# Block attention and two gated layers on one core: value sums copied in three pieces, C21 activated first, and masking with its maximum as one VectorE operation per head pair

## The chip, the cores and the metric

The kernel runs on one core of a Trainium2 chip. Five engines work side by side, each on its own list of instructions in order, and wait for one another on semaphores: TensorE (PE, matmuls into the accumulation memory, `ps`), VectorE (DVE), ScalarE (ACT), GpSimd (POOL) and SyncE (SP, which here only issues DMAs). DMAs are issued on two queues, one of SP (q1 in the profile) and one of ACT (q10). The metric is the device time of one execution in microseconds; lower is better.

## The reference, cut to what matters

Attention over 2 batches, 8 heads, 768 positions, head width 64. A query sees the keys less than 16 positions away, and beside them 24 summaries, one for every block of 32 keys; the attention output goes through a gated layer and then a second layer.

```
k_sum = k by blocks of 32: maximum;   v_sum = v by blocks of 32: mean
scores_l = scale * q k^T,  -1e9 where |i - j| >= 16
scores_s = scale * q k_sum^T + log(32)
a = softmax over [scores_l, scores_s];  x = a @ [v, v_sum]
g = x @ w_gate;  y = (g * sigmoid(g) * (x @ w_val)) @ w_out
h = y @ w_in;    out = where(h >= 1, h, where(h <= -1, 0, (h + 1)^2 / 4)) @ w_out2
```

## The kernel before, in words

**Attention tiles.** Queries are handled in 24 tiles `s` of 64 positions, 12 of each batch. A tile takes all 8 heads as 4 head pairs, 128 partitions (64 positions of each of two heads) by 128 columns a pair: 96 keys in and around the tile, 24 summaries, 8 columns of padding. For each tile:

- PE: `scores(s)` (L486).
- DVE: `mask_scores(s)`: a first instruction (L1050) reads the scores of all four pairs from `ps`, 128x512, multiplies by the scale, adds the mask and writes `masked`. A second one (L1053) reads `masked` back and writes the four negated maxima to `neg_max`. Between the two it waits for its own semaphore `masked_ready`; ACT waits for the second (`max_ready`).
- ACT: `exponentials(s)` (L773): one activation for each head pair, with the negated maximum as bias, and the row sum as a second output, which shows in the profile as an instruction of its own (ACTIVATION_READ_ACCUMULATOR).
- DVE: `inverses(s)` (L1059, L1061); POOL: `normalise(s)` (L1335); PE: `transposes` (L493); ACT: `copy_trans` (L784); PE: `values` (L514), whose right operand `v_s` has 96 rows of values and under them 32 rows of value sums; the result is copied to `raw` by DVE (first batch, `first_copy_out`, L1065) or ACT (second batch).

**The first batch** (`LAST_A` = 12 tiles, up to about 57 us) runs as a pipeline: at step `s` PE does the scores of `s`, the transposes of `s-3` and the values of `s-7` (`VLAG`). At steps 3 to 5 it also makes the value sums (L471), which ACT copies to `v_sum` (L749). `place_first_sums` then puts them under the values of all 12 tiles: tiles 0 and 1 by one activation (L752), tiles 2 to 11 by one DMA on ACT's queue (L755, 640 KB). PE waits for that DMA (`v_first_sums`) before the values of tile 2. The values themselves, the keys of the second batch (`k_raw_b`) and weights come on SP's queue at the same time. DVE also makes the low part of weight unit 0: `w_lo_a(0)` and `w_lo_b(0)` (L1115, L1125) at step 1 and `w_lo_s(0)` (L1120) at step 4.

**The second batch's 12 tiles** are woven into phase 0 of the layers, one tile for each unit `u` (about 70 to 175 us).

**The layers.** Each product is done in three matmuls of high and low parts (L524), with the matrix cut 2x2 and seven block products a unit; `c11`, `c12`, `c21`, `c22` are the blocks of the result. In phases 0 and 1 even units are gates, odd ones values. For a gate, ACT takes C21 out of `ps` to `silu[:, 3]` (L871), then `silu_c11` (L879), and `silu_rest`: first blocks 1 and 2 in one activation (L883, after `c12_ready` of DVE), then C21 (L885). The value unit's `h21` on DVE (L1151) multiplies C21 and frees the bank for the first product (`p1`) of the unit after next; POOL multiplies the other blocks (L1345). Phases 2 and 3 are the second layer.

**Order.** Nothing is scheduled by a planner: each engine's order is the order of the calls in the code.

Of the kernel before, what the change touches and what calls it, by code (L numbers as in the profile page):

```python
# [9 lines left out]
ACT = mybir.ActivationFunctionType  # L10
ALU = mybir.AluOpType
AX = mybir.AxisListType

P = 128
B, H, S, D = 2, 8, 768, 64
BLOCK, WINDOW = 32, 16
SCALE = 1.0 / math.sqrt(D)
MASKED = -1e9
DM = H * D
TOK = B * S  # L20
KD = DM // P
PAIRS = H // 2

QT = 64
TILES = S // QT
G = B * TILES
SUB = 16
WIN = QT + 2 * WINDOW
NB = S // BLOCK
COLS = 128  # L30
# [5 lines left out]
RING = 4  # L36
# [31 lines left out]
LAST_A = G // 2  # L68
FIRST = TILES // 2
VLAG = 7  # L70

def phase_of(u):
# [31 lines left out]
def build(nc, q_t, k_t, v_rows, w1, w2, out):  # L105
    ctx = ExitStack()
    with ctx:
# [3 lines left out]
        def sem(name):  # L111
            return ctx.enter_context(nc.semaphore(name))
# [14 lines left out]
        part = at("part", 112640, [2, 3, T])  # L127
        silu = at("silu", 121856, [4, T])
# [3 lines left out]
        v_s = at("v_s", 128000, [TILES, DM])  # L132
# [14 lines left out]
        v_sum = at("v_sum", 193536, [B, DM])  # L147
        masked = at("masked", 197632, [2, PAIRS, COLS])
# [3 lines left out]
        mask = at("mask", 207872, [2 * MASKS, COLS])  # L152
        ident = at("ident", 210944, [P])
        k_sum = at("k_sum", 211456, [B, 2, PAIRS, SUB])
        neg_max = at("neg_max", 212480, [RING, PAIRS])
# [16 lines left out]
        def score_banks(s):  # L172
            b = 0 if s < LAST_A and s % 2 == 0 else AT0
            return ps[:, b:b + 2, 0:2 * COLS]
# [45 lines left out]
        def prob_of(s):  # L220
            return prob_s[:, s % RING] if s < LAST_A else prob[:, s % 2]
# [16 lines left out]
        qk_loaded = [sem(f"qk_loaded{j}") for j in range(6)]  # L238
        v_first_loaded = [sem(f"v_first_loaded{j}") for j in range(FIRST)]
        v_pair_sums = sem("v_pair_sums")  # L240
        v_first_sums = sem("v_first_sums")
        v_late_loaded = [sem(f"v_late_loaded{j}") for j in range(2)]
        v_late_sums = [sem(f"v_late_sums{j}") for j in range(2)]
        scores_done = sem("scores_done")
        masked_ready = sem("masked_ready")
        max_ready = sem("max_ready")
        exp_done = sem("exp_done")
        denom_ready = sem("denom_ready")
        inv_ready = sem("inv_ready")
# [32 lines left out]
        c21_act = sem("c21_act")  # L282
        c21_dve = sem("c21_dve")
        silu_c11_ready = sem("silu_c11_ready")
        silu_ready = sem("silu_ready")
        h_pool = sem("h_pool")

# [174 lines left out]
        def _(pe):  # L462
# [33 lines left out]
            def values(s, dst):  # L496
                v, c0 = v_slots(s // 2)
                r = c0 + s % 2
                if s % 2 == 0:
                    pr = s // 2  # L500
                    pe.wait_ge(v_first_loaded[pr] if pr < FIRST else v_late_loaded[pr % 2], v_count(pr))
                    if s == 0:
                        pe.wait_ge(v_pair_sums, 1)
                    elif s == 2:
                        pe.wait_ge(v_first_sums, 16)
                    if pr in (FIRST, FIRST + 1):
                        pe.wait_ge(v_late_sums[pr % 2], 16)
                pe.wait_ge(prob_t_ready, s + 1)
                for x in range(2):
                    for half, row in ((0, 0), (1, 1), (1, 0), (0, 1)):  # L510
                        i = 2 * row + x
                        a = pair_at(i, half)
                        c = (2 * a + row) * D
                        last = nc.tensor.matmul(dst[row * D:row * D + D, a], v[:, r, c:c + D],  # L514
                                                prob_t_of(s)[:, i, half * QT:half * QT + QT], start=True, stop=True)
                last.then_inc(attn_done, 1)
# [184 lines left out]
            for k in range(PHASES):  # L701
                u1 = PH_U0[k] + PH_LEN[k] - 1
                for r in range(PH_LEN[k]):
                    u = PH_U0[k] + r
# [41 lines left out]
        def _(act):  # L746
# [4 lines left out]
            def place_first_sums():  # L751
                nc.scalar.activation(v_s[WIN:, 0:2], v_sum_ps[0][WIN:, :].unsqueeze(1).to_broadcast([P - WIN, 2, DM]),  # L752
                                     ACT.Copy).then_inc(v_pair_sums, 1)
                act.wait_ge(v_sum_ready, 1)
                act.dma_start(v_s[WIN:, 2:], v_sum[WIN:, 0].unsqueeze(1).to_broadcast([P - WIN, TILES - 2, DM])  # L755
                              ).then_inc(v_first_sums, 16)

            def place_late_sums(j):
                act.wait_ge(v_sum_ready, 2)
# [2 lines left out]
                              ).then_inc(v_late_sums[j], 16)  # L762

            def exponentials(s):
                act.wait_ge(max_ready, s + 1)
                if s < LAST_A:
                    if s >= RING:
                        act.wait_ge(trans_done, s - RING + 1)
                elif s >= LAST_A + 2:
                    act.wait_ge(trans_done, s - 1)  # L770
                c = s % RING
                for a in range(PAIRS):
                    last = nc.scalar.activation(prob_of(s)[:, a], masked[:, s % 2, a], ACT.Exp,  # L773
                                                bias=neg_max[:, c, a:a + 1], accum_out=total[:, c, a:a + 1])
                last.then_inc(exp_done, 1)

# [102 lines left out]
                nc.scalar.activation(silu[:, 0], part[:, u % 2, 0], ACT.Silu).then_inc(silu_c11_ready, 1)  # L879

            def silu_rest(u):
                act.wait_ge(c12_ready, u + 1)
                nc.scalar.activation(silu[:, 1:3], part[:, u % 2, 1:3], ACT.Silu)  # L883
                act.wait_ge(c21_act, u // 2 + 1)
                nc.scalar.activation(silu[:, 3], silu[:, 3], ACT.Silu).then_inc(silu_ready, 1)  # L885

            def wout_part_hi(k, i):
# [142 lines left out]
        def _(dve):  # L1031
# [10 lines left out]
            def mask_scores(s):  # L1042
                t = s % TILES
                m = 0 if t == 0 else MASKS - 1 if t == TILES - 1 else 1
                dve.wait_ge(scores_done, s + 1)
                if s >= 2:
                    dve.wait_ge(exp_done, s - 1)
                rows = mask[:, 2 * m:2 * m + 2].rearrange("p x c -> p (x c)").unsqueeze(1)
                rows = rows.to_broadcast([P, 2, 2 * COLS])
                nc.vector.scalar_tensor_tensor(masked[:, s % 2].rearrange("p (b x) c -> p b (x c)", b=2), score_banks(s),  # L1050
                                               SCALE, rows, ALU.mult, ALU.add).then_inc(masked_ready, 1)
                dve.wait_ge(masked_ready, s + 1)
                nc.vector.tensor_reduce(neg_max[:, s % RING], masked[:, s % 2], AX.X, ALU.max, negate=True  # L1053
                                        ).then_inc(max_ready, 1)

            def inverses(s):
                c = s % RING
# [89 lines left out]

            def h21(u):
                dve.wait_ge(p4_done, u + 1)
                dve.wait_ge(silu_ready, u // 2 + 1)  # L1150
                nc.vector.tensor_tensor(h[:, chunks_of(u)[1], 0:T], x_ps(u), silu[:, 3], ALU.mult).then_inc(c21_dve, 1)  # L1151

# [34 lines left out]
            for j in range(P // BLOCK):  # L1188
                last = nc.vector.memset(sel[j * BLOCK:(j + 1) * BLOCK, SEL0 + j:SEL0 + j + 1], 1.0 / BLOCK)
            last.then_inc(sel_ready, 1)  # L1190
            nc.vector.memset(mask[:, :, WIN:WIN + NB], math.log(BLOCK))
            nc.vector.memset(mask[:, :, WIN + NB:], MASKED)
            nc.vector.memset(half[:], 0.5).then_inc(half_ready, 1)
            nc.vector.memset(k_sum[:, :, 1, :, NB - SUB:], 0.0).then_inc(pads_ready, 1)
# [10 lines left out]
            for s in range(LAST_A):  # L1205
                mask_scores(s)
                if s >= 1:
                    inverses(s - 1)
                if s > VLAG:
                    first_copy_out(s - VLAG - 1)  # L1210
                if s == 1:
                    w_lo_a(0)
                    w_lo_b(0)
                elif s == 4:
                    w_lo_s(0)
# [194 lines left out]
```

## Time and profile before

| | us |
|---|---|
| median of three runs | 624.05 (623.77 to 625.68) |
| profiled execution, its own time | 624.35 |
| its span, first to last instruction | 622.5 |
| PE busy in the span | 588.6 (95%) |
| DVE busy | 479.6 (77%) |
| ACT busy | 365.0 (59%) |
| mean granted TensorE clock | 0.994 |

The span is what the trace shows; the 1.85 us by which the execution's time exceeds it lie around it. PE is busy nine tenths or more of nearly every fortieth from the sixth on; the forty slices show it idle in the first four or five (2, 9, 5, 8, 8 tenths), which are the first batch's attention. So this is a kernel bound by PE for most of its length, with a short first stage in which PE waits.

### The profile page before, as it was taken

What the parts mean: (1) busy time and instruction counts of PE and PEld (TensorE: products, weight loads), DVE (VectorE), ACT (ScalarE), POOL (GpSimd) and SP (SyncE); (2) the same over time, 40 slices, a digit from 0 to 9 for tenths busy, and PEclk for the clock granted to TensorE, in tenths of its full rate; (3) what the DMA queues carried; (4) which work ended last, traced back from release to release, by engine and by line L of the source; (5) the groups of instructions that cost most, each with busy time, mean ns of one, the idle gap of its engine ahead of it and who ended that gap; (6) DMA issues with size and microseconds to landing.
All of it is one profiled execution on the core that took longest, in us unless ns stands there. A gap on an engine that the chain in (4) does not pass through costs nothing.

```text
span 622.5 us, 10059 instructions
## 1 busy us (share of the span) xinstructions
PE 588.6 (95%) x3720; PEld 538.7 (87%) x3720; DVE 479.6 (77%) x770; ACT 365.0 (59%) x735; POOL 87.2 (14%) x78
## 2 busy tenths in 40 slices
PE   2958889999999999999999999999999999999997
PEld 2436679888889999999999999999878899998886
DVE  6649698899858656888867756997998569979843
ACT  3845687887865536555554536666565356665532
POOL 4425032324330001222320000000000000000000
PEclk9979999999999999999999999999999999999999
DMA  9968333425112211223222112322212233012212
GB/s 332 308 180 274 99 111 119 131 66 187 35 53 74 63 34 41 93 72 102 85 68 70 51 35 69 113 74 68 68 52 67 102 103 97 23 35 67 68 51 102
DMA packets 32928, 59.77 MB, mean 96 GB/s; under 512 B 3248, under 2 KB 7344, under 8 KB 32880
## 3 DMA queue, kind: packets, MB, share of 16 engines
q1 hardware_dynamic: 32384, 58.21, 29.3%
q10 hardware_dynamic: 496, 0.92, 0.6%
q8 instruction: 30, 0.49, 0.3%
q14 instruction: 18, 0.15, 0.1%
HBM read 54.53 MB, written 3.15 MB: 93 GB/s over the span
## 4 chain that ended last, share of the span: by engine, by line
PE 73%; DVE 13%; ACT 5%; issue 4%; DMA 3%; POOL 1%; SPq 0%; ACTq 0%; POOLq 0%; DVEq 0%
PE ps L524 38%; PE ps L661 17%; PE ps L633 15%; DMA v_s<-v_sum 2%; PE ps L486 1%; ACT prob L773 1%; DVE hid_lo L1163 1%; ACT L879 1%; DVE masked L1050 1%; DVE w_sum L1107 1%; DVE w_sum L1109 1%; DMA k_a<-k_t_dram 1%; PE ps L493 1%; DVE rel L1169 1%; PE ps L471 1%
## 5 line engine op out<-in xcount | busy, mean ns | idle before, releaser
L524 PE MATMUL ps<-x_hi,w_hi 128*128 128x384 f32 x560 | 191.2, 341 | 5.7 <-DVE h L1151 3.1
L524 PE MATMUL ps<-x_lo,w_hi 128*128 128x384 f32 x560 | 187.4, 335 | 0.0
L524 PE MATMUL ps<-x_hi,w_lo 128*128 128x384 f32 x560 | 187.2, 334 | 0.0
L524 PEld LDWEIGHTS ps<-x_hi,w_hi 128*128 128x128 f32 x560 | 105.1, 188 | 10.2 <-issue 4.9
L524 PEld LDWEIGHTS ps<-x_hi,w_lo 128*128 128x128 f32 x560 | 105.2, 188 | 0.4 <-issue 0.2
L524 PEld LDWEIGHTS ps<-x_lo,w_hi 128*128 128x128 f32 x560 | 105.1, 188 | 0.0
L893 ACT ACTIVATE wout_hi<-wout_raw 128x512 fp32r<-128x512 f32 x56 | 35.3, 631 | 95.1 <-PE ps L661 52.0
L661 PE MATMUL ps<-wout_hi,hid_hi 128*128 128x512 f32 x192 | 74.8, 389 | 0.8 <-DVE wout_lo L1157 0.8
L661 PE MATMUL ps<-wout_hi,hid_lo 128*128 128x512 f32 x192 | 75.2, 392 | 0.1
L661 PE MATMUL ps<-wout_lo,hid_hi 128*128 128x512 f32 x192 | 74.8, 390 | 0.0
L1157 DVE TENSOR_TENSOR wout_lo<-wout_raw,wout_hi 128x512 fp32r<-128x512 f32 x56 | 39.4, 704 | 40.1 <-ACT wout_hi L893 39.6
L1345 POOL TENSOR_TENSOR h<-part,silu 128x384 f32<-128x384 f32 x36 | 47.7, 1333 | 138.1 <-ACT silu L885 90.6
L633 PE MATMUL ps<-hid_lo,wout_hi 128*128 128x384 f32 x192 | 64.5, 336 | 0.6 <-DVE hid_lo L1163 0.6
L633 PE MATMUL ps<-hid_hi,wout_hi 128*128 128x384 f32 x192 | 64.3, 335 | 0.7 <-DVE wout_lo L1157 0.7
L633 PE MATMUL ps<-hid_hi,wout_lo 128*128 128x384 f32 x192 | 64.1, 334 | 0.0
L1120 DVE TENSOR_TENSOR w_lo<-w_sum,w_hi 128x1024 fp32r<-128x1024 f32 x40 | 48.8, 1220 | 19.3 <-ACT w_hi L829 19.3
L1163 DVE TENSOR_TENSOR hid_lo<-h,hid_hi 128x768 fp32r<-128x768 f32 x56 | 53.5, 956 | 1.4
L906 ACT ACTIVATE hid_hi<-h 128x768 fp32r<-128x768 f32 x56 | 46.6, 832 | 2.4 <-DVE h L1172 2.4
L829 ACT ACTIVATE w_hi<-w_sum 128x1024 fp32r<-128x1024 f32 x40 | 42.2, 1055 | 7.4 <-PE ps L524 5.1
L661 PEld LDWEIGHTS ps<-wout_hi,hid_lo 128*128 128x128 f32 x192 | 36.0, 188 | 8.5 <-DVE hid_lo L1163 1.2
L661 PEld LDWEIGHTS ps<-wout_hi,hid_hi 128*128 128x128 f32 x192 | 36.0, 188 | 8.4 <-issue 1.1
L661 PEld LDWEIGHTS ps<-wout_lo,hid_hi 128*128 128x128 f32 x192 | 36.0, 188 | 7.5
(105 smaller groups left out, 920.1 us busy)
## 6 DMA issues: line engine op xcount, KB each, us to landing
w_raw<-w_dram SPq DMA_DIRECT2D x80, 256.0 KB, 2.9
wout_raw<-w_dram SPq DMA_DIRECT2D x56, 256.0 KB, 2.6
out_dram<-y_out SPq DMA_DIRECT2D x12, 256.0 KB, 2.1
k_a<-k_t_dram SPq DMA_DIRECT2D x6, 384.0 KB, 6.8
v_s<-v_rows_dram SPq DMA_DIRECT2D x6, 384.0 KB, 14.8
v_a<-v_rows_dram SPq DMA_DIRECT2D x6, 384.0 KB, 3.7
k_raw<-k_t_dram SPq DMA_DIRECT2D x3, 512.0 KB, 4.5
q_a<-q_t_dram SPq DMA_DIRECT2D x6, 256.0 KB, 6.5
```

The lines of the kernel that those rows point to most:

```text
L471: last = nc.tensor.matmul(v_sum_ps[b][:], sel[:, c0:c0 + P], v_tok[b][:, i], start=i == 0, stop=i == VCH - 1)
L486: last = nc.tensor.matmul(dst[half * QT:half * QT + QT, row, x * COLS:x * COLS + COLS], q[rows, r, a], k[rows, r, :, a], start=True, stop= ...
L524: last = nc.tensor.matmul(dst, lhs, rhs, start=start and kk == 0 and i == 0, stop=kk == 1 and i == 2, skip_group_check=not start)
L633: last = nc.tensor.matmul(bank[ACC1[j]][:, 0:T], lhs, rhs, start=i == 0 and e == 0, stop=ends and e == 2)
L661: last = nc.tensor.matmul(bank[ACC2[j]][:], lhs, rhs, start=i == 0 and e == 0, stop=ends and e == 2)
L829: nc.scalar.activation(w_hi[:, u % 2, W_S2:W_S4 + 1], w_sum[:], ACT.Copy).then_inc(ws_hi, 1)
L893: nc.scalar.activation(wout_hi[:, n % 2], wout_raw[:, n % RAWS], ACT.Copy).then_inc(wout_hi_ready, 1)
L906: nc.scalar.activation(hid_hi[:, n % 2], h[:, c], ACT.Copy).then_inc(hid_hi_ready, 1)
L1120: nc.vector.tensor_tensor(w_lo[:, u % 2, W_S2:W_S4 + 1], w_sum[:], w_hi[:, u % 2, W_S2:W_S4 + 1], ALU.subtract).then_inc(ws_lo, 1)
L1157: nc.vector.tensor_tensor(wout_lo[:, n % 2], wout_raw[:, n % RAWS], wout_hi[:, n % 2], ALU.subtract).then_inc(wout_lo_ready, 1)
L1163: nc.vector.tensor_tensor(hid_lo[:, n % 2], h[:, c], hid_hi[:, n % 2], ALU.subtract).then_inc(hid_lo_ready, 1)
L1345: nc.gpsimd.tensor_tensor(dst, part[:, u % 2, c], silu[:, c], ALU.mult).then_inc(h_pool, 1)
```

## The change

Four edits:

1. `place_first_sums` issues three DMAs in place of one: tiles 2 and 3, tiles 4 to 7, tiles 8 to 11 (128, 256 and 256 KB), each with its own semaphore. PE waits for the first before the values of tile 2, for the second before those of tile 4, for the third before those of tile 8.
2. `mask_scores` does for each of the four head pairs one `tensor_tensor_reduce` of 128x128: (score + mask) times minus the scale, written to `masked`, and its minimum to `neg_max` as a second output. `masked` is thus negated, the exponential takes it with scale -1, and the mask's log(32) is divided by the scale. `max_ready` is gone; ACT waits for `masked_ready`, which now comes after the last pair.
3. `silu_rest` activates C21 first, with a semaphore of its own (`silu_c21_ready`) that `h21` waits for; then blocks 1 and 2.
4. `w_lo_a(0)` and `w_lo_b(0)` stand at step 3 in place of step 1.

```diff
+SUMS_AT = ((2, 4), (4, 8), (8, TILES))
@@ values, on PE
-                    elif s == 2:
-                        pe.wait_ge(v_first_sums, 16)
+                    for j, (c0, _) in enumerate(SUMS_AT):
+                        if s == c0:
+                            pe.wait_ge(v_first_sums[j], 16)
@@ place_first_sums, on ACT
-                act.dma_start(v_s[WIN:, 2:], v_sum[WIN:, 0].unsqueeze(1).to_broadcast([P - WIN, TILES - 2, DM])
-                              ).then_inc(v_first_sums, 16)
+                for j, (c0, c1) in enumerate(SUMS_AT):
+                    act.dma_start(v_s[WIN:, c0:c1], v_sum[WIN:, 0].unsqueeze(1).to_broadcast([P - WIN, c1 - c0, DM])
+                                  ).then_inc(v_first_sums[j], 16)
@@ exponentials, on ACT
-                act.wait_ge(max_ready, s + 1)
+                act.wait_ge(masked_ready, s + 1)
-                    last = nc.scalar.activation(prob_of(s)[:, a], masked[:, s % 2, a], ACT.Exp,
+                    last = nc.scalar.activation(prob_of(s)[:, a], masked[:, s % 2, a], ACT.Exp, scale=-1.0,
@@ silu_rest, on ACT
+                act.wait_ge(c21_act, u // 2 + 1)
+                nc.scalar.activation(silu[:, 3], silu[:, 3], ACT.Silu).then_inc(silu_c21_ready, 1)
                 act.wait_ge(c12_ready, u + 1)
-                nc.scalar.activation(silu[:, 1:3], part[:, u % 2, 1:3], ACT.Silu)
-                act.wait_ge(c21_act, u // 2 + 1)
-                nc.scalar.activation(silu[:, 3], silu[:, 3], ACT.Silu).then_inc(silu_ready, 1)
+                nc.scalar.activation(silu[:, 1:3], part[:, u % 2, 1:3], ACT.Silu).then_inc(silu_ready, 1)
@@ mask_scores, on DVE
-                rows = mask[:, 2 * m:2 * m + 2].rearrange("p x c -> p (x c)").unsqueeze(1)
-                rows = rows.to_broadcast([P, 2, 2 * COLS])
-                nc.vector.scalar_tensor_tensor(masked[:, s % 2].rearrange("p (b x) c -> p b (x c)", b=2), score_banks(s),
-                                               SCALE, rows, ALU.mult, ALU.add).then_inc(masked_ready, 1)
-                dve.wait_ge(masked_ready, s + 1)
-                nc.vector.tensor_reduce(neg_max[:, s % RING], masked[:, s % 2], AX.X, ALU.max, negate=True
-                                        ).then_inc(max_ready, 1)
+                rows = mask[:, 2 * m:2 * m + 2]
+                for i in range(PAIRS):
+                    last = nc.vector.tensor_tensor_reduce(
+                        masked[:, s % 2, i], score_banks(s)[:, i // 2, i % 2 * COLS:i % 2 * COLS + COLS], rows[:, i % 2],
+                        -SCALE, 3e38, ALU.add, ALU.min, neg_max[:, s % RING, i:i + 1])
+                last.then_inc(masked_ready, 1)
@@ h21, on DVE
-                dve.wait_ge(silu_ready, u // 2 + 1)
+                dve.wait_ge(silu_c21_ready, u // 2 + 1)
@@ on DVE, before the tiles
-            nc.vector.memset(mask[:, :, WIN:WIN + NB], math.log(BLOCK))
+            nc.vector.memset(mask[:, :, WIN:WIN + NB], math.log(BLOCK) / SCALE)
@@ the first batch's steps, on DVE
-                if s == 1:
+                if s == 3:
                     w_lo_a(0)
                     w_lo_b(0)
```

DVE, steps 1 and 2 of the first batch, before (masking of tile 1, inverses of tile 0, low weight parts, masking of tile 2, with what each waits for):

```order
L1050 SCALAR_TENSOR_TENSOR masked<-ps,mask 128x512 [waits scores_done]
L1053 TENSOR_REDUCE neg_max<-masked 128x4 [waits masked_ready]
L1059 TENSOR_SCALAR denom<-total 128x4 [waits exp_done]
L1061 RECIPROCAL inv<-denom 128x4 [waits denom_ready]
L1115 TENSOR_TENSOR w_lo<-w_raw,w_hi 128x512 [waits wa_hi]
L1125 TENSOR_TENSOR w_lo<-w_raw,w_hi 128x256 [waits wb_hi]
L1050 SCALAR_TENSOR_TENSOR masked<-ps,mask 128x512 [waits exp_done,scores_done]
```

DVE, the same place now: the inverses of tile 0, the masking of tile 2, and the inverses of tile 1:

```order
L1061 TENSOR_SCALAR denom<-total 128x4 [waits exp_done]
L1063 RECIPROCAL inv<-denom 128x4 [waits denom_ready]
L1053 ISA masked,neg_max<-ps,mask 128x128 [waits exp_done,scores_done]
L1053 ISA neg_max 128x1
L1053 ISA masked,neg_max<-ps,mask 128x128
L1053 ISA neg_max 128x1
...
L1061 TENSOR_SCALAR denom<-total 128x4 [waits exp_done]
L1063 RECIPROCAL inv<-denom 128x4 [waits denom_ready]
```

A tile's masking, two instructions before, is eight now: four of 128x128 and behind each one that writes its second output, 128x1. None of the eight waits for DVE itself. The two `w_lo` instructions stand two steps later.

ACT at steps 5 and 6, before (copy of the value sums, their placing under tiles 0 and 1, the DMA for tiles 2 to 11, then the copy of tile 3's transposes and the exponentials of tile 6):

```order
L749 ACTIVATE v_sum<-ps 32x512 [waits v_sum_done]
L752 ACTIVATE v_s<-ps 32x1024
L755 DMA v_s<-v_sum 32x10x512 [waits v_sum_ready]
L784 ACTIVATE prob_ts<-ps 128x512 [waits trans_done]
L773 ACTIVATE prob_s,total<-masked,neg_max 128x128 [waits trans_done,max_ready]
```

ACT, the same place now:

```order
L751 ACTIVATE v_sum<-ps 32x512 [waits v_sum_done]
L754 ACTIVATE v_s<-ps 32x1024
L758 DMA v_s<-v_sum 32x2x512 [waits v_sum_ready]
L758 DMA v_s<-v_sum 32x4x512 x2
L787 ACTIVATE prob_ts<-ps 128x512 [waits trans_done]
L776 ACTIVATE prob_s,total<-masked,neg_max 128x128 [waits trans_done,masked_ready]
```

Three issues stand where one did, ahead of everything that ACT does for the tiles from 3 on; the rest of its order is the same up to the gates' `silu_rest`.

## Rows read from the trace of the kernel before

**Rows 1.** The page: PE's busy tenths in 40 slices, and the chain that ended last.

```profile
PE   2958889999999999999999999999999999999997
...
PE 73%; DVE 13%; ACT 5%; issue 4%; DMA 3%; POOL 1%; SPq 0%; ACTq 0%; POOLq 0%; DVEq 0%
```

**Rows 2.** Stretches: us, busy of PE, PEld, DVE, ACT, POOL, PEclk, DMA share, GB/s.

```profile
33.70:41.10 7.40, 0.00 (x0) 0.03 (x1) 1.46 (x5) 2.83 (x14) 1.37 (x2) 0.76 0.99 283
41.10:44.30 3.20, 3.20 (x38) 2.42 (x38) 0.92 (x2) 0.00 (x0) 0.00 (x0) 0.50 0.04 18
...
47.90:62.00 14.10, 12.71 (x145) 8.66 (x143) 13.96 (x23) 6.61 (x18) 8.05 (x7) 1.00 0.92 296
```

**Rows 3.** PE in time order: start, us, line, out<-in, count, idle before.

```profile
31.59 0.69 PE L514 MATMUL ps<-prob_ts,v_s 128*64 128x64 f32 x16
32.21 0.67 PE L486 MATMUL ps<-k_a,q_a 64*64 64x128 f32 x16
33.03 0.66 PE L493 MATMUL ps<-ident,prob_s 128*128 128x128 f32 x4 [0.15 <-ACT prob_ts L784]
41.10 1.12 PE L514 MATMUL ps<-prob_ts,v_s 128*64 128x64 f32 x16 [7.42 <-DMA v_s<-v_sum]
```

**Rows 4.** ACT's DMA queue from 31.4 to 33.4 us; the DMA's size and landing.

```profile
q10 hardware_dynamic: 37, 0.08, 16.7%
...
v_s<-v_sum ACTq DMA_DIRECT2D x1, 640.0 KB, 13.4
```

**Rows 5.** ACT in time order, 27 to 68 us.

```profile
27.44 0.72 ACTq L755 DMA_DIRECT2D v_s<-v_sum  x1
...
36.33 0.20 ACT L773 ACTIVATION_READ_ACCUMULATOR prob_s<-masked,neg_max 128x1 f32 x1
44.36 0.60 ACT L784 ACTIVATE prob_ts<-ps 128x512 f32<-128x512 f32 x1 [7.83 <-PE ps L493]
...
67.52 0.49 ACT L859 ACTIVATE part<-ps 128x384 f32<-128x384 f32 x1 [1.38 <-issue]
```

**Rows 6.** The second batch's keys: issues (ns, first and last start), and landing.

```profile
L340 SPq DMA_DIRECT2D k_raw_b<-k_t_dram x3: 515/734/1120, 22.4 to 24.2; - x3
...
DMA to landing us min/median/max: 18.2/18.3/18.9
```

**Rows 7.** DVE in time order, first batch: a copy, the masking behind it, key maxima.

```profile
32.83 0.39 DVE L1065 COPY raw<-ps 128x256 f32<-128x256 f32 x1
33.14 0.68 DVE L1050 SCALAR_TENSOR_TENSOR masked<-ps,mask 128x512 f32<-128x512 f32 x1
...
47.93 1.21 DVE L1035 TENSOR_REDUCE k_sum<-k_raw_b 128x32 f32<-128x1024 f32 x1
```

**Rows 8.** ACT in time order: an exponential, the read of its sum, the next.

```profile
29.22 0.39 ACT L773 ACTIVATE prob_s<-masked,neg_max 128x128 f32<-128x128 f32 x1
29.51 0.19 ACT L773 ACTIVATION_READ_ACCUMULATOR prob_s<-masked,neg_max 128x1 f32 x1
29.61 0.39 ACT L773 ACTIVATE prob_s<-masked,neg_max 128x128 f32<-128x128 f32 x1
```

**Rows 9.** POOL in time order: the normalisations of tiles 0 and 1.

```profile
13.69 1.40 POOL L1335 TENSOR_TENSOR prob_s<-prob_s,inv 128x512 f32<-128x512 f32 x1 [0.59 <-DVE inv L1061]
17.06 1.04 POOL L1335 TENSOR_TENSOR prob_s<-prob_s,inv 128x512 f32<-128x512 f32 x1 [1.97 <-DVE inv L1061]
```

**Rows 10.** DVE in time order, in phase 0: masking, low weight part, h21.

```profile
107.12 0.67 DVE L1050 SCALAR_TENSOR_TENSOR masked<-ps,mask 128x512 f32<-128x512 f32 x1
107.83 0.69 DVE L1053 TENSOR_REDUCE neg_max<-masked 128x4 f32<-128x512 f32 x1
108.43 0.68 DVE L1115 TENSOR_TENSOR w_lo<-w_raw,w_hi 128x512 fp32r<-128x512 f32 x1
109.03 0.55 DVE L1151 TENSOR_TENSOR h<-ps,silu 128x384 f32<-128x384 f32 x1
```

**Rows 11.** Who waited for whom, 75 to 220 us: total us, times, longest.

```profile
PE ps L524 <- DVE h L1151: 3.1, 5, 0.9
```

More of the change, by code:

```diff
@@ L240, in build @@
         v_pair_sums = sem("v_pair_sums")
-        v_first_sums = sem("v_first_sums")
+        v_first_sums = [sem(f"v_first_sums{j}") for j in range(len(SUMS_AT))]
         v_late_loaded = [sem(f"v_late_loaded{j}") for j in range(2)]
@@ L245, in build @@
         masked_ready = sem("masked_ready")
-        max_ready = sem("max_ready")
         exp_done = sem("exp_done")
@@ L284, in build @@
         silu_c11_ready = sem("silu_c11_ready")
+        silu_c21_ready = sem("silu_c21_ready")
         silu_ready = sem("silu_ready")
```

## The prediction

> **What bounds the kernel now.** I read the page's forty slices and chain first, then the stretches, then PE's, ACT's and DVE's rows in time order around the edits, and last the waits. The chain is PE for 73% of the span, and PE is nine tenths busy or more in every slice from the seventh to the last but one [rows 1]. There an edit on another engine can hardly gain. What the change can move lies in the first batch's attention, in the slices before, and in phase 0 as far as PE waits there.
>
> The one large hole: PE would start the values of tile 2 behind the transposes at 33.03 + 0.66 = 33.7 us, and starts them at 41.10, after 7.42 us of waiting for the DMA of the value sums [rows 3]. ACT has nothing to do from 36.5 to 44.36 us [rows 5]. The wait hurts twice: the granted clock is 0.50, TensorE's lower level of 1.2 GHz, for the 3.2 us behind it, after an engine that had been idle [rows 2].
>
> **Three pieces.** The DMA is issued at 27.44 [rows 5] and takes 13.4 us to land, to 40.85 [rows 4]. Until 33.4 us its queue has moved 37 packets, 0.08 of the 0.64 MB, all behind 31.4 [rows 4]; an eighth of the way is done at 33.4, so the first packets leave at some 32.5, and the whole takes 8.4 us beside SP's transfers. Ahead of the first piece's end lie only its own bytes, a fifth: 32.5 + 0.2 x 8.4 = 34.2, and up to a microsecond for the slowest of 16 engines and the semaphore. I take 35.2. The second piece ends at three fifths, about 38, the third at about 41.
>
> What it adds: two issues on ACT, ahead of all that ACT does from tile 3 on. The two later issues of this kind held ACT up for 1.38 us with work behind them [rows 5]; I take 1.3. From there to 36.5 us ACT has nearly no gap, and PE waits for ACT's copies (0.15 us ahead of the transposes at 33.03 [rows 3]), so PE comes to the values of tile 2 at up to 34.9 in place of 33.7. That lies inside the wait for the piece. The values start at R = 35.2.
>
> What is late next is ACT itself. Its exponentials of tile 9 end at 36.5 [rows 5], now at 37.8. The transposes that it needs then are ready 0.69 + 0.67 + 0.66 us behind R at full clock [rows 3], at 37.2. So its copy starts at 37.8 in place of 44.36 [rows 5], 6.55 us sooner. From there to tile 11 a few tenths of waiting for PE at half clock and for DVE go too: 6.7 in all. A tile costs ACT four times 0.39 [rows 8] and a copy of 0.60 [rows 5], about 2 us, so tile 4's values are wanted at R + 4 = 39 and tile 8's behind 43: neither waits for its piece.
>
> Then DVE's copies and key maxima. The first maxima start at 47.93 [rows 7], now at 41.2. Their keys, issued from 22.4 on, take 18.3 us: the first third is there at 40.7, the last at 24.2 + 18.9 = 43.1 [rows 6]. The cover is half a microsecond. From 47.9 to 62 us DVE is busy 13.96 of 14.1 us [rows 2], so that stretch just moves forward. Term: **-6.7 us**, with ends -7.4 (the whole wait) and -4 (pieces or keys late, below).
>
> **Low weight parts two steps later.** At step 1 they stood ahead of tile 2's masking and beside POOL's first normalisation, which took 1.40 us against the next one's 1.04 [rows 9], and PE's first transposes wait for it. They hide behind DVE's wait for scores at step 4; without that cover they cost what they cost before. PE's chain starts up to 0.36 us earlier, which does not reach the landing of the piece if SP's backlog sets that. Between 0 and -0.36: **-0.1**.
>
> **Masking.** Before: two instructions, 1.31 us from the start of the masking to the start of what follows (107.12 to 108.43) [rows 10]. Now four of 128x128 out of `ps` and four that write a second output. No row shows either. A copy of 128x256 out of `ps` takes 0.31 us start to start [rows 7], a reduction of 128x512 0.60 [rows 10]; the line through them gives 0.165 for 128 columns, and by the durations, 0.39 and 0.69, it gives 0.24. The nearest row for a second output is ACT's: the read starts 0.29 us behind the exponential, the next exponential 0.10 behind the read, so a pair takes no longer than the exponential's own duration, 0.39 [rows 8]. Carried over: 0.24 a pair, 0.97 a tile. If the read costs its 0.19 whole on top of 0.165, it is 1.42 a tile; if nothing overlaps (0.24 + 0.19), 1.7; with a free read, 0.66. I take 1.2, between the two middle readings: 0.1 less than before.
>
> The Trainium skill, VectorE: DVE Perf Modes, Rules for kernel authors, speaks against this edit: chained operations should not be fused for speed, the number of operations should be kept down. Here the columns read are halved and two instructions become eight, so by that rule the tile would get slower and by the estimate a little faster; no row of before decides it.
>
> It counts where PE waits for DVE. In phase 0 PE waits five times, 3.1 us in all, 0.9 once and so 0.55 each otherwise, for `h21` [rows 11], which stands right behind masking and `w_lo` [rows 10]. A tenth less on DVE is a tenth less on PE in six pairs of units: **-0.6 us**, with ends -2.7 (free read: of 3.1 nearly all) and +6 (1.7 a tile, in the way of the third rival). In the first batch DVE's tile hides behind ACT's 2 us. `masked_ready` comes later for PE than before, at the end of all four pairs, but PE asks for it a step later: nothing.
>
> **C21 first.** `h21` stands on DVE behind masking and `w_lo`, when C21 is long activated, so PE's waits for it [rows 11] end on DVE's own order. In phase 1 there are none of them in the list, and PE's work hides what ACT gains: **0**.
>
> **Sum.** -6.7 - 0.1 - 0.6 = -7.4 on the profiled execution: span 622.5 to 615.1, and with the 1.85 us around it 624.35 to 616.95. It lies 0.3 above the median of the runs, so 624.05 - 7.4 = **616.65 us**. A difference within 0.3% (1.9 us) is called no change, about what a measurement of this kernel can tell.
>
> **Rivals.** *The next transfer takes the wait's place.* The first piece or the keys land late, since the 16 DMA engines are 0.99 busy [rows 2]. At R = 38 ACT's copy starts at 40, 4.4 us sooner, and the sum is about -5: 619.1. For it: half a microsecond of cover at the keys. Against: bytes and order are the same.
>
> *The second output is nearly free.* 0.66 to 0.97 a tile, 0.65 to 0.34 less than before in six pairs, as far as there is wait to take: -2 to -2.7 in place of -0.6, 614.5 to 615.3. For it: ACT's pair takes no longer than its exponential [rows 8].
>
> *The second output drains the engine.* This is the other side: a pair takes 0.6 us, 2.4 a tile, 1.1 more than before. Phase 0 pays it in each of six pairs of units ahead of `h21`, and again ahead of the next exponentials, which start the other tile's way to DVE: 12 x 1.1 = 13.2. In the first batch DVE's tile (2.4 + 0.31 for a copy, and the inverses) passes ACT's 2 us, some +3 from tile 8 on. 624.05 - 6.8 + 16.2 = 633.5. It eats half the gain from 0.38 us a pair on and turns the sign at about 0.45. Against: that is nearly twice a 128-column duration.
>
> *The change doesn't do what it says.* The three pieces land together at 41. Then the wait stays and hides ACT's two issues: 623.5. Against: the pieces have a semaphore each and follow one another on one queue.
>
> **How the numbers follow.** Forecast 0.62 (615.3 to 618). Late transfers 0.15 (618 to 621). Nearly free output 0.13 (614.5 to 615.3). Dear output 0.07, of which 0.04 slower than before. No use of the pieces 0.03. The range, 614.6 to 620.6, leaves out the ends of these, under 2 in 10. Faster 0.92, no change 0.04, slower 0.04.
>
> **What would show it.** PE's wait for `v_s` between 33 and 41 us shrinks to under 2 us, and the granted clock stays at 2.4 GHz behind it. ACT shows three issues and then runs without a gap to tile 11. The second batch's first key maxima start at about 41. In phase 0 PE's waits for `h21` shrink by a tenth each, and a tile's eight instructions take 1.0 to 1.4 us. It would be wrong if the key maxima start after 43, or if the eight take over 1.6 us.

## The result and the profile after

```
                          before   after
median of the runs, us    624.87   614.01   (after 613.82 to 615.82, 4 runs; before 623.77 to 626.07)
profiled execution, us             614.17
span, us                  622.5    612.4
first key maxima, us       47.93    41.10
first h21, us              89.72    81.47
a pair of units, us        19.31    18.84
```

The ratio is 0.9832, with an interval of 0.9803 to 0.9861. The prediction was 616.65 us, range 614.6 to 620.6; the time lies 2.6 us under it and 0.6 us under the range.

The page of the kernel after, first PE's and the clock's slices and the chain, which answer to [rows 1]:

```profile
PE   2889999999999999999999999999999999999997
...
PEclk9989999999999999999999999999999999999999
...
PE 80%; DVE 9%; SPq 3%; DMA 3%; issue 2%; ACT 2%; POOL 0%; ACTq 0%; POOLq 0%; DVEq 0%
```

PE is 80% of the chain instead of 73%. The 5 in its third slice has gone, and the row of nines begins in the fourth slice instead of the seventh. DMA still has 3%, now by the second batch's keys.

PE in time order at the start of the first batch (start, us, line, out<-in, count, idle before), which answers to [rows 3]:

```profile
28.42 1.12 PE L494 MATMUL ps<-ident,prob_s 128*128 128x128 f32 x4 [2.36 <-ACT prob_ts L787]
29.46 1.12 PE L516 MATMUL ps<-prob_ts,v_s 128*64 128x64 f32 x16
...
34.72 0.66 PE L494 MATMUL ps<-ident,prob_s 128*128 128x128 f32 x4
35.30 0.69 PE L516 MATMUL ps<-prob_ts,v_s 128*64 128x64 f32 x16
```

No row here waits for `v_s`. The values of tile 2 start at 35.30 us, not 41.10. But PE waited 2.36 us for ACT at 28.42, and from there its groups take 1.12 us instead of 0.66 to 0.69. The stretches show the clock (us, busy of PE, PEld, DVE, ACT, POOL, PEclk, DMA share, GB/s), and answer to [rows 2]:

```profile
27.40:34.20 6.80, 5.78 (x68) 4.56 (x72) 1.85 (x13) 5.62 (x24) 2.08 (x2) 0.53 1.07 265
34.20:41.10 6.90, 6.40 (x122) 4.80 (x116) 5.01 (x35) 6.35 (x30) 3.12 (x3) 0.97 1.05 298
41.10:55.20 14.10, 12.48 (x139) 8.42 (x135) 13.96 (x22) 6.24 (x16) 7.46 (x6) 1.00 0.94 307
```

Over 6.8 us the mean granted clock is 0.53, so nearly all of the stretch is at the lower level of 1.2 GHz (0.50). Ahead of it stood the 2.36 us without work. What PE waited for shows on ACT, in time order, which answers to [rows 5], and in the landing of the three pieces, which answers to [rows 4]:

```profile
25.37 2.35 ACTq L758 DMA_DIRECT2D v_s<-v_sum  x3
27.77 0.60 ACT L787 ACTIVATE prob_ts<-ps 128x512 f32<-128x512 f32 x1 [1.52 <-issue]
...
35.41 0.60 ACT L787 ACTIVATE prob_ts<-ps 128x512 f32<-128x512 f32 x1 [0.55 <-PE ps L494]
...
DMA to landing us min/median/max: 8.0/9.4/10.4
```

The three issues hold ACT for 2.35 us. The first piece, issued at 25.37, is there 8.0 us later, at 33.4. By then the values of tile 2 are still behind the slow groups on PE, so nobody waits for it. The DVE rows of the second batch's keys answer to [rows 7]:

```profile
41.10 1.22 DVE L1038 TENSOR_REDUCE k_sum<-k_raw_b 128x32 f32<-128x1024 f32 x1 [0.48 <-DMA k_raw_b<-k_t_dram]
...
42.86 1.19 DVE L1038 TENSOR_REDUCE k_sum<-k_raw_b 128x32 f32<-128x1024 f32 x1
...
47.22 1.20 DVE L1038 TENSOR_REDUCE k_sum<-k_raw_b 128x32 f32<-128x1024 f32 x1
```

```profile
80.02 0.28 DVE L1053 CUSTOM_DVE_ANT_0 masked<-ps,mask 128x128 f32<-128x128 f32 x1
80.23 0.08 DVE L1053 DVE_READ_ACCUMULATOR2_ANT neg_max<- 128x1 f32 x1
80.23 0.28 DVE L1053 CUSTOM_DVE_ANT_0 masked<-ps,mask 128x128 f32<-128x128 f32 x1
...
80.86 0.08 DVE L1053 DVE_READ_ACCUMULATOR2_ANT neg_max<- 128x1 f32 x1
80.86 0.68 DVE L1117 TENSOR_TENSOR w_lo<-w_raw,w_hi 128x512 fp32r<-128x512 f32 x1
81.47 0.55 DVE L1153 TENSOR_TENSOR h<-ps,silu 128x384 f32<-128x384 f32 x1
```

The read starts together with the next operation, each operation 0.21 us behind the last, and `w_lo` starts 0.84 us behind the masking. Before it was 1.31. The waits from 60 to 220 us (total us, times, longest), which answer to [rows 11]:

```profile
PE ps L526 <- ACT part L862: 1.4, 1, 1.4
PE ps L494 <- POOL prob L1337: 1.0, 1, 1.0
PE ps L635 <- DVE wout_lo L1159: 0.7, 1, 0.7
PE ps L526 <- DVE h L1153: 0.4, 1, 0.4
```

PE's waits for `h21` are down from 3.1 us in five to 0.4 in one.

**Where the 10.1 us of the span went.** Up to the first key maxima: 47.93 to 41.10, 6.83 us. From there to the first `h21`: 41.79 before, 40.37 after, 1.42 us. Over the four pairs of units that follow: 4 x 0.47 = 1.9 us. Together 10.1. And 1.42 is three times 0.47, the 1.31 - 0.84 of a tile: three tiles of the second batch are masked in this stretch, and in the kernel before PE waited for DVE behind each (the last row is the first of the five waits of [rows 11]):

```profile
72.79 0.41 PE L524 MATMUL ps<-x_hi,w_hi 128*128 128x384 f32 x1 [0.33 <-DVE part L1140]
...
79.48 0.44 PE L524 MATMUL ps<-x_hi,w_hi 128*128 128x384 f32 x1 [0.26 <-DVE w_lo L1115]
...
90.42 0.41 PE L524 MATMUL ps<-x_hi,w_hi 128*128 128x384 f32 x1 [0.92 <-DVE h L1151]
```

Two of these waits are shorter than 0.47 us, but the stretches between the same groups of PE bear the figure out. From 68.16 to 76.12, 82.87 and 90.42 it is 7.96, 6.75 and 7.55 us; in the kernel after, from 61.31 to 68.81, 75.08 and 82.16, it is 7.50, 6.27 and 7.08. Each is 0.46 to 0.48 us shorter. So seven tiles stand on PE's path, at 0.47 us each: 3.3 us. PE's waits say the same: 3.1 + 0.3 + 0.3 us before, 0.4 now.

### The profile page after: what moved, and what is told of

The parts are those of the page before. It is cut to its first block, busy times and chain, and to the rows that moved or that the text cites. A ratio compares the mean times of both kernels' runs of the same rounds, so it can differ in the third digit from the quotient of the medians.

```text
span 612.4 us, 10207 instructions
## 1 busy us (share of the span) xinstructions
PE 588.3 (96%) x3720; PEld 539.3 (88%) x3720; DVE 469.8 (77%) x914; ACT 365.1 (60%) x735; POOL 87.2 (14%) x78
## 4 chain that ended last, share of the span: by engine, by line
PE 80%; DVE 9%; SPq 3%; DMA 3%; issue 2%; ACT 2%; POOL 0%; ACTq 0%; POOLq 0%; DVEq 0%
PE ps L526 45%; PE ps L663 17%; PE ps L635 15%; DMA k_raw_b<-k_t_dram 3%; DVE hid_lo L1165 1%; SPq L380 1%; PE ps L516 1%; PE ps L487 1%; DVE rel L1171 1%; DVE x_lo L1097 1%; DVE h L1174 1%; SPq L359 1%; PE ps L494 1%; DVE t_first L1089 1%; DVE t_late L1089 1%
```

## Experiments

The times are medians in us; the ratios are against runs of the kernel before that were taken on the same chip in between.

```
kernel                   median  ratio   95% interval      span   first key  h21 waits
before                    624.9                            622.5   47.93     3.1, 5
after                     614.01 0.9832  0.9803 to 0.9861  612.4   41.10     0.4, 1
only pieces               618.26 0.9895  0.9882 to 0.9907  616.1   41.51     3.1, 5
only two-output masking   620.24 0.9922  0.9906 to 0.9937  618.8   47.46     0.4, 1
only C21 first            624.77 0.9998  0.9990 to 1.0007  623.3   48.65     3.1, 5
only w_lo later           623.79 0.9984  0.9975 to 0.9993  622.5   47.87     3.1, 5
after without pieces      619.09 0.9902  0.9882 to 0.9922  617.2   45.97     0.4, 1
after, masking of before  618.12 0.9886  0.9866 to 0.9906  616.2   41.69     3.1, 5
after, w_lo at step 1     614.10 0.9828  0.9813 to 0.9843  613.0   41.67     0.4, 1
after + DVE work          616.96 0.9874  0.9861 to 0.9888  614.5   40.67     2.5, 5
after, pieces later       614.77 0.9835  0.9822 to 0.9849  613.2   41.27     0.4, 1
same, keys first          612.86 0.9810  0.9797 to 0.9824  611.3   40.09     0.4, 1
after, keys first         613.76 0.9814  0.9790 to 0.9837  611.9   40.18     0.4, 1
```

### Each part alone

The diffs below are cut to the main lines of each edit.

**Three pieces only**, on the kernel before:

```diff
-                act.dma_start(v_s[WIN:, 2:], v_sum...).then_inc(v_first_sums, 16)
+                for j, (c0, c1) in enumerate(SUMS_AT):
+                    act.dma_start(v_s[WIN:, c0:c1], v_sum...).then_inc(v_first_sums[j], 16)
```

> The kernel before with the value sums in three pieces alone. Theory (the pieces give the first-stage term, masking gives the rest): the pieces are issued at 27.4 us, ACT is held up 1.3 to 1.5 us, tile 2's values start at about 35.3 to 36, the second batch's first key maxima at 41.2 to 42 in place of 47.9: 6.0 to 6.8 us less than before, and PE's waits for h21 in phase 0 stay at about 3.1 us. Rival (the pieces gain more than the rest lets be seen): 7.4 or more less.

618.26 us, 6.4 us off the span. The key maxima start at 41.51, and the `h21` waits are those of before. The pieces' term holds in size. PE's wait behind ACT's issues is there too (2.76 us ahead of the transposes at 30.10, and 1.12 us for the values behind; the kernel before has 1.27 us at this place), so it belongs to the pieces.

**Two-output masking only**, on the kernel before:

```diff
-                nc.vector.scalar_tensor_tensor(masked..., score_banks(s), SCALE, rows, ALU.mult, ALU.add)
-                nc.vector.tensor_reduce(neg_max..., masked..., AX.X, ALU.max, negate=True)
+                for i in range(PAIRS):
+                    last = nc.vector.tensor_tensor_reduce(masked..., score_banks(s)..., rows[:, i % 2],
+                        -SCALE, 3e38, ALU.add, ALU.min, neg_max[:, s % RING, i:i + 1])
```

> The kernel before with the masking as four two-output operations a tile alone. Theory (masking was mis-sized): a tile's masking takes 0.84 us in place of 1.31, PE's wait for h21 in phase 0 goes from 3.1 to under 0.6 us, and the time falls by 3 to 3.5 us; the wait for the value sums stays at about 7 us, a little longer since PE gets there sooner. Rival (C21 first is what ended the waits for h21): less than 1 us gained, waits for h21 still near 3.

620.24 us: the ratio gives 4.9 us (3.9 to 5.9), the span 3.7. Of the span 0.47 came ahead of the key maxima; from the maxima to the first `h21` (87.84) it is 40.38 us as in the kernel after, against 41.79. This is the part that the prediction put at 0.6. It is more than the 3 to 3.5 us expected here by the median, and close to it by the span; the six runs lie 3.6 us apart (618.38 to 621.95). PE's waits for `h21` fell to 0.4 us without C21 being first, which rules out the rival.

**C21 first only**:

```diff
-                act.wait_ge(c12_ready, u + 1)
-                nc.scalar.activation(silu[:, 1:3], part[:, u % 2, 1:3], ACT.Silu)
                 act.wait_ge(c21_act, u // 2 + 1)
-                nc.scalar.activation(silu[:, 3], silu[:, 3], ACT.Silu).then_inc(silu_ready, 1)
+                nc.scalar.activation(silu[:, 3], silu[:, 3], ACT.Silu).then_inc(silu_c21_ready, 1)
+                act.wait_ge(c12_ready, u + 1)
+                nc.scalar.activation(silu[:, 1:3], part[:, u % 2, 1:3], ACT.Silu).then_inc(silu_ready, 1)
```

> The kernel before with C21 activated first alone. Theory: no change, within 0.5 us, waits of PE for h21 near 3.1 us. Rival (C21 first ends the waits for h21): 2 to 3 us less.

624.77 us, a ratio of 0.9998, and the same `h21` waits. Nothing, as predicted. The key maxima of the profiled execution came 0.7 us later, with some 10.2 us at the lower clock around the end of the wait for the sums instead of 6.8 (from the mean granted clock of windows there); the edit is not at work there, and the median shows none of it.

**Low weight parts later only**:

```diff
-                if s == 1:
+                if s == 3:
```

> The kernel before with the low weight parts of unit 0 at step 3 alone. Theory: the value sums' DMA is issued 0.4 to 1.5 us sooner, and this is lost in the wait for it: 0 to 0.7 us less than before. Rival (the move is worth the 2 us by which the issue came sooner in the changed kernel): 1.5 to 2 us less.

623.79 us, 1.0 us less (0.4 to 1.6) by the ratio, a little more than the 0 to 0.7 expected, and an equal span. The DMA is issued at 26.38 instead of 27.44, and PE's wait for it ends at 40.20 instead of 41.10. In the profiled execution that gain was used up at once: PE's groups kept the lower clock until about 46 us instead of 44.3, and the key maxima started at 47.87. The four parts alone give 6.4 + 3.7 - 0.8 + 0 = 9.3 us of span; together they gave 10.1.

### One part taken out of the changed kernel

**One transfer instead of three** (the first diff, reversed):

> The changed kernel with one transfer for the value sums of tiles 2 to the end, and all else of the change kept. Theory (the first transfer's landing at 40.9 sets the values of tile 2, whatever else stands ahead of it): PE waits some 7.4 us for the sums again, the second batch's first key maxima start at 47.3 to 47.9, and the kernel takes 619.4 to 620.6 us, 5.5 to 6.8 over the changed kernel. Rival (issuing earlier, since w_lo is out of the way, lands the one transfer earlier): key maxima at 46 to 47 and 618.5.

619.09 us, span 4.8 above the kernel after. The wait for the sums is back, 7.26 us, but it ends at 39.61 and not 41.10:

```profile
39.61 1.12 PE L514 MATMUL ps<-prob_ts,v_s 128*64 128x64 f32 x16 [7.26 <-DMA v_s<-v_sum]
```

The transfer was issued at 26.11 and not 27.44, and the key maxima started at 45.97. The rival was right on the landing and, within 0.03 us, on the key maxima; the time lies between the rival's 618.5 and the theory's 619.4. The wait ended 1.5 us earlier with an issue 1.3 us earlier. The other single transfers say the same (issued at 27.27, 27.21 and 26.38, waits ended at 40.95, 40.98 and 40.20), so the landing followed the issue. In the kernel after the pieces are worth less (4.8) than alone (6.4).

**The masking of before** (the second diff, reversed):

> The changed kernel with the masking of before (one instruction and one reduction a tile) and all else of the change kept. Theory (the two-output form is worth about 0.47 us on DVE in each of phase 0's pairs of units, plus the waits for w_lo and part behind it): PE's waits for h21 are back at 3.1 us, the pair period is back at 19.3 us, the first key maxima start at 41.1 to 41.6, and the kernel takes 617.0 to 618.2 us. Rival (the term of the prediction, 0.6 us): 614.6. Second rival (the form is worth what it is worth alone before the other edits, 4.9 us): 618.9.

618.12 us, inside the expected range, and the key maxima at 41.69, a tenth behind it. The span is 3.8 above: 0.59 ahead of the key maxima, 1.41 to the first `h21` (83.47), the rest in the pairs. C21 is still activated first here, and yet all three waits of PE for DVE are back:

```profile
PE ps L527 <- DVE h L1155: 3.1, 5, 0.9
...
PE ps L527 <- DVE part L1144: 0.3, 1, 0.3
PE ps L527 <- DVE w_lo L1119: 0.3, 1, 0.3
```

**Low weight parts back at step 1** (the fourth diff, reversed):

> The changed kernel with the low weight parts of unit 0 back at step 1. Theory (their gain in the start chain is swallowed by the wait for the second batch's keys, 0.48 us, and by ACT): the value sums are issued about 1 us later than in the changed kernel, the first key maxima start at 41.1 to 41.6, 0 to 0.5 us slower. Rival (the move is worth what it brought the issue forward): 1 us slower or more.

614.10 us: not to be told from 614.01. The pieces are issued at 26.69. DVE waited 0.87 us for the keys at 41.67 instead of 0.48 at 41.10.

### More work on DVE ahead of h21

If DVE's time ahead of `h21` is what counts, added time must come out again, seven times:

```diff
             def mask_scores(s):
+                if s >= LAST_A:
+                    dve.wait_ge(masked_ready, s)
+                    nc.vector.memset(v_sum[:, 0, 0:390], 0.0)
```

> The changed kernel with one more DVE instruction (a fill of 128x390 in memory that nothing reads any more, 0.47 us by the trace's rate) ahead of each of the second batch's 12 maskings, so that a tile costs DVE there what it did before. It gives 0.84 + 0.47 = 1.31 us. Theory (phase 0's gain is DVE's time ahead of h21 and nothing else): the pair period returns from 18.84 to 19.31 us, PE's waits for h21 return to about 3 us, 3.3 us slower than the changed kernel, 617.3. Rival (the gain came from the self-wait that went, or from C21 first): under 1 us slower.

The fill cost less than expected. DVE in time order:

```profile
79.83 0.54 DVE L1139 TENSOR_TENSOR part<-ps,part 128x384 f32<-128x384 f32 x1
80.40 0.38 DVE L1053 MEMSET v_sum<- 128x390 f32 x1
80.71 0.22 DVE L1056 CUSTOM_DVE_ANT_0 masked<-ps,mask 128x128 f32<-128x128 f32 x1
...
81.50 0.68 DVE L1120 TENSOR_TENSOR w_lo<-w_raw,w_hi 128x512 fp32r<-128x512 f32 x1
82.10 0.54 DVE L1156 TENSOR_TENSOR h<-ps,silu 128x384 f32<-128x384 f32 x1
```

From `part` to `h21` it is 2.27 us, and 1.92 in the kernel after (79.55 to 81.47): 0.35 more a tile. The pair of units takes 19.21 us instead of 18.84, 0.37 more, and from the key maxima to the first `h21` (82.10) it is 41.43, 1.06 or three times 0.35 more. The span rose by 2.1 = 1.06 + 4 x 0.37 - 0.43 (the key maxima started sooner), the median by 2.9, against 3.3 expected of a fill of 0.47 us. A tenth of a microsecond on DVE here is a tenth on PE, in seven places.

### What bounds the first stage now

**Pieces 2 and 3 issued later**, behind the exponentials of tiles 6 and 7:

```diff
                     place_first_sums()
+                elif s in (6, 7):
+                    place_piece(s - 5)
```

> The changed kernel with the second and third piece issued by ACT after the exponentials of tiles 6 and 7, in place of at once. Theory (after the pieces, ACT's stall of 1.5 us and the low clock behind PE's 2.4 us of idling are the cost, but the second batch's keys cap the gain): PE's idle time before the transposes of tile 4 falls from 2.4 to about 1.2 us, the first key maxima still start at 41.1 since their keys land then, the wait for them grows from 0.5 to 1.5 us or more, and the time stays within 0.5 us of the changed kernel. Rival (ACT is the bound there): 1.3 us less or more.

The key maxima still wait for their keys, as the theory has it. PE's rows show what took the place of its wait for ACT:

```profile
28.28 0.65 PE L494 MATMUL ps<-ident,prob_s 128*128 128x128 f32 x4 [0.86 <-ACT prob_ts L790]
...
32.31 0.66 PE L494 MATMUL ps<-ident,prob_s 128*128 128x128 f32 x4
34.98 0.69 PE L516 MATMUL ps<-prob_ts,v_s 128*64 128x64 f32 x16 [2.02 <-DMA v_s<-v_sum]
```

PE's wait for ACT fell from 2.36 to 0.86 us and its groups took 0.65 to 0.69 us. It then waited 2.02 us for the first piece and went on at 34.98, where the kernel after is at 35.30. The key maxima waited 1.19 us for their keys, at 41.27. 614.77 us: no gain. By the median it is 0.8 us more than the kernel after, where no more than 0.5 was expected, by the ratio 0.2 us, which the intervals do not settle.

Here the first piece was issued at 26.72, 1.35 us later than in the kernel after. In the next version, with the same late pieces, it was issued at 25.45 like in the kernel after, and PE went on with the values of tile 2 at 33.79. So ACT's issues and the low clock did cost the kernel after some 1.5 us at that point, 35.30 against 33.79; the wait for the keys behind it took this up.

**The same with the keys first** (the same edit in the loads, on SP's queue):

```diff
+            for c in range(3):
+                load_k_raw(1, c)
             load_v(4)
             load_v(5)
-            for c in range(3):
-                load_k_raw(1, c)
```

> As b3_later, and the second batch's keys are loaded ahead of the values of tiles 8 to 11. Theory (keys were the cap): the keys land near 38 us, the first key maxima start at 38.5 to 39.5, 1.5 to 2.5 us less than the changed kernel, unless the values of tile 8, now landing near 42, are waited for. Rival (the cap is elsewhere, DVE's own row of work): within 0.5 us of the changed kernel.

> The changed kernel with one edit: the second batch's keys are loaded ahead of the values of head pairs 4 and 5, the three pieces issued together as in the changed kernel. Theory (the keys are the cap of the first stage by half a microsecond): the wait of 0.48 us ahead of the second batch's first key maxima goes, these start at 40.3 to 40.7 instead of 41.10, and the kernel takes 613.2 to 613.8 us, 0.3 to 0.8 under the changed kernel. Rival (the gain of the version with both edits comes from issuing pieces 2 and 3 later): no change here, 614.0, and a wait for values of pair 4 shows up. Second rival: the two edits are worth the same together as this one alone, 612.9.

The first of these texts is for this edit with later pieces, the second for this edit alone. The loads of the values of pairs 4 and 5 go behind those of `k_raw_b`. With later pieces: 612.86 us, 1.9 less than without the keys moved, the key maxima at 40.09 with no wait (38.5 to 39.5 was expected). Without later pieces: 613.76, the maxima at 40.18 with no wait, but the third of them at 46.79, only 0.43 sooner than in the kernel after, and PE now waited 1.2 us for one of DVE's copies. Against the kernel after that is 1.2 and 0.25 us, both less than expected. The two are not told apart, since their intervals lie over each other. With the keys there, the maxima follow DVE's other work without a gap. In the version with later pieces that work had itself waited 1.63 us for PE's scores, up to 38.30 and behind a slow group of PE; so in that version PE's chain, slow groups included, sets the maxima. The version with both edits has the lowest median of all kernels run. It is clearly faster than the kernel before; against the kernel after its ratio is 0.002 lower, which the intervals do not settle.

## Why the prediction missed

**The step that failed** is the masking term: "I take 1.2, between the two middle readings: 0.1 less than before", and "a tenth less on PE in six pairs of units: -0.6 us". Both factors were off. A tile takes 0.84 us, 0.47 less than before. And the places are seven, not six, since PE also waited once for `part` and once for `w_lo` behind a masking, which the list of `h21` waits did not have. 7 x 0.47 = 3.3 in place of 0.6: this is the 2.7 us by which the span fell below its forecast of 615.1. That the first batch hides the masking wholly is not shown either: the two masking runs have 0.47 and 0.59 us ahead of the key maxima, each in one profile, and the issue times of the pieces scatter by more than that.

What went wrong in it can be read from the choice. By the nearest row for a second output, ACT's [rows 8], the prediction had carried over a pair that takes no longer than the operation's own duration: 0.24, 0.97 a tile. DVE does still better, 0.21 start to start at a duration of 0.285, and its read starts with the next operation instead of 0.10 ahead of it. The 1.2 was a mean of 0.97 and 1.42, and no mechanism gave 1.2; it was given the highest chance all the same. The rival "the second output is nearly free" (0.66 to 0.97 a tile, 614.5 to 615.3, chance 0.13) is the case that came. Even it fell half a microsecond high, by the waits that its cap of 3.1 us left out.

Where the 0.47 comes from inside DVE is only argued. The second pass over 512 columns, which read `masked` back, is gone, and the reads of the second output lie beside the next operation; no run has the operation without that output. A part, some 0.13 us by estimate, is DVE's wait for itself, which is gone: [rows 10] have the reduction starting 0.04 us behind the masking's end, and `w_lo` 0.09 ahead of the reduction's end.

The Trainium skill, VectorE: DVE Perf Modes, Rules for kernel authors, advises against fusing chained operations for speed, and asks for a small number of operations. The trace disagrees: here eight short instructions took 0.47 us less a tile than two long ones, 0.84 against 1.31.

**Pieces** (-6.7): 6.8 in the kernel after up to the first key maxima, which takes in what the other edits give there; 6.4 alone, and 4.8 as the last edit, where the one transfer too is issued earlier. The size was right, the way to it only in part. The first piece was there at 33.4, 1.8 us sooner than R = 35.2, since it was issued 2.07 us earlier; from its issue it took 8.0 us, and the forecast had 7.8. What held the values of tile 2 until 35.30 was ACT's issues, 2.35 us of them instead of the one, and the clock behind the idle PE. That "the granted clock stays at 2.4 GHz behind it" came true at 35.30 only after 6.8 us at the lower clock ahead of it, and that ACT "then runs without a gap to tile 11" was wrong: it waited 0.82 us at 32.73 and 0.55 at 35.41. The key maxima came within a tenth of the forecast, 41.10 for 41.2, and there the half microsecond of cover was used up, to a wait of 0.48. That is luck in part: the forecast had the chain of ACT reach that point, and it was the keys that set it. For the same reason later issues alone brought nothing.

**Low weight parts** (-0.1): the reasoning that an earlier issue does not reach the landing was wrong. The first piece was there 8.0 us after an issue at 25.37 and 8.0 after one at 26.72; the one transfer 13.4 us after 27.44 and 13.3 after 26.11. The landing followed the issue. Yet in the changed kernel the edit is worth 0.1 us in the median, since the keys take what it gives. How much of the 2.07 us is due to this edit stays open: kernels with the same code on ACT up to there issued at 25.37, 25.45, 26.02, 26.60 and 26.72, so one profile does not tell a microsecond here.

**C21 first** (0): 0, alone and by the run with the masking of before, where it left all the waits for `h21` in place.

**Rivals.** No late transfer (a wait of 0.48 us for keys is all), no dear second output, and the three pieces did not land together (8.0, 9.4 and 10.4 us after their issues).

## What to carry to other kernels

Price an operation that no row shows by the mechanism that has the nearest row, here another engine's read of a second output, and let a value between two mechanisms stand only as a bound. Multiply a change on an engine by the places where its whole order is waited for, by any tile, and not only by the waits for the one result that was looked at. And where a wait of seven microseconds goes, look for the next arrival: with the second batch's keys landing half a microsecond after DVE was ready for them, nothing more was to be had from the sums until the keys were loaded earlier.

## What the hardware did that was not expected

- The two-output operation over 128x128 out of `ps`: 285 ns long, 0.21 us start to start, its read (82 ns) beside the next operation, 96 of each:

```profile
L1053 DVE CUSTOM_DVE_ANT_0 masked<-ps,mask 128x128 f32<-128x128 f32 x96 | 22.0, 285 | 10.2 <-PE ps L487 10.2
L1053 DVE DVE_READ_ACCUMULATOR2_ANT neg_max<- 128x1 f32 x96 | 7.9, 82 | 0.0
```

- PE's clock after an idle time: 2.36 and 2.76 us without work stood ahead of low-clock groups (1.12 us instead of 0.66 to 0.69) in the kernel after and in the one with pieces only; 0.86 did not. The length of the idle time does not settle it. With more DVE work, 2.34 us of it was followed by a group at full speed and only then by slow ones:

```profile
29.63 0.66 PE L494 MATMUL ps<-ident,prob_s 128*128 128x128 f32 x4 [2.34 <-ACT prob_ts L787]
30.21 0.80 PE L516 MATMUL ps<-prob_ts,v_s 128*64 128x64 f32 x16
30.94 1.13 PE L487 MATMUL ps<-k_a,q_a 64*64 64x128 f32 x16
```

A wait of 2.02 us was followed by full speed in the kernel with later pieces, and one of 2.10 us, in that with the keys first too, by slow groups from 35.01:

```profile
33.79 0.69 PE L516 MATMUL ps<-prob_ts,v_s 128*64 128x64 f32 x16 [2.10 <-DMA v_s<-v_sum]
34.40 0.67 PE L487 MATMUL ps<-k_a,q_a 64*64 64x128 f32 x16
35.01 1.11 PE L494 MATMUL ps<-ident,prob_s 128*128 128x128 f32 x4
36.05 1.12 PE L516 MATMUL ps<-prob_ts,v_s 128*64 128x64 f32 x16
```

- Three DMA issues on ACT in a row held it for 2.35 us, 0.61 to 0.72 each and the gaps between them, when its next copy was what PE waited for.
- A fill of 128x390 took 0.38 us on DVE, and the masking behind it began 0.31 us after its start.
